# Query and key projections moved behind other small products on TensorE, and the features of block 2 built by square transposes and DMA

## What is computed

```python
def phi(x):                                  # r = 8: 64 features of a head's 32 channels
    a = np.einsum('rd,bhsd->bhsr', S1, x)
    b = np.einsum('rd,bhsd->bhsr', S2, x)
    return np.einsum('bhsi,bhsj->bhsij', a, b).reshape(*x.shape[:-1], r * r)
...
kv = np.einsum('bhsf,bhsd->bhfd', phi(k), v)         # q, k, v: (4, 4, 1088, 32)
num = np.einsum('bhsf,bhfd->bhsd', phi(q), kv)
den = np.einsum('bhsf,bhf->bhs', phi(q), z)[..., None] + 1e-06
x = num / den                                # as (4352 tokens, 128)
xn = x / rms(x) * rms_g
y = (silu(xn @ w_gate) * (xn @ w_val)) @ w_out       # d_ff = 1536
...                                          # then a soft mixture of 8 experts over y:
logits = y @ phi                             # softmax over the tokens gives 32 slots,
                                             # w1, relu, w2 on the slots, softmax over the
                                             # slots mixes them back into the tokens
```

## Time and profile before

| | |
|---|---|
| median of the runs | 303.69 us (303.5 to 303.74) |
| the profiled execution | 304.61 us, of which its span is 301.8 us |
| PE busy | 288.5 us, 96% of the span |
| DVE busy | 228.5 us, 76% |
| ACT busy | 159.1 us, 53% |
| DMA | 25.09 MB in 61040 packets, 45649 of them under 512 B |

### The profile page before, as it was taken

One profiled execution on the slowest core, in us unless ns is written; L12 is line 12 of the kernel. 1 busy time (PEld: TensorE's weight loads), 2 busy tenths in 40 slices (PEclk: granted clock), 3 DMA queues, 4 the chain that ended last, 5 costly groups with the idle time before them and its releaser, 6 DMA issues.

```text
span 301.8 us, 6603 instructions
## 1 busy us (share of the span) xinstructions
PE 288.5 (96%) x2551; PEld 234.3 (78%) x2551; DVE 228.5 (76%) x440; ACT 159.1 (53%) x302; POOL 30.2 (10%) x50
## 2 busy tenths in 40 slices
PE   7799999999999989999999999999999999999983
PEld 6687787888787868888878788888788878797572
DVE  4746877886998797988788979797778668865423
ACT  1475654635556446347564473456456556547421
POOL 1168001000100010003200100020000003000000
PEclk9999999999999999999999999999999999999995
DMA  6999200000203123233112201972199310010017
GB/s 184 330 238 244 72 2 1 2 0 2 72 13 51 28 33 47 32 88 51 26 27 39 32 9 26 346 253 42 25 284 293 50 28 13 13 24 3 0 39 261
DMA packets 61040, 25.09 MB, mean 83 GB/s; under 512 B 45649, under 2 KB 57682, under 8 KB 61010
## 3 DMA queue, kind: packets, MB, share of 16 engines
q1 hardware_dynamic: 60722, 24.38, 31.9%
q10 hardware_dynamic: 288, 0.30, 0.3%
HBM read 17.45 MB, written 2.23 MB: 65 GB/s over the span
## 4 chain that ended last, share of the span: by engine, by line
PE 76%; DVE 10%; DMA 4%; ACT 3%; issue 3%; SPq 2%; DVEq 0%; ACTq 0%
PE bank L1006 73%; DMA area<-in_moe_w_out 4%; DVE hid L851 3%; DVE hl L857 2%; PE bank L1086 1%; ACT silu L578 1%; SPq L349 1%; DVE area L789 1%; DVE area L998 1%; DVE area L768 1%; DVE area L810 1%; DVE ssq L800 1%; ACT woh L627 1%; PE bank L1047 0%; DVE area L744 0%
## 5 line engine op out<-in xcount | busy, mean ns | idle before, releaser
L851 DVE TENSOR_TENSOR hid<-bank,silu 128x512 f32<-128x512 f32 (+1 forms) x108 | 70.8, 656 | 43.2 <-PE bank L1006 22.7
L578 ACT ACTIVATE silu<-bank 128x512 f32<-128x512 f32 (+1 forms) x108 | 61.8, 573 | 73.0 <-PE bank L1006 72.2
L857 DVE TENSOR_TENSOR hl<-hid,hh 128x512 fp32r<-128x512 f32 (+1 forms) x108 | 70.8, 655 | 0.0
L586 ACT ACTIVATE hh<-hid 128x512 fp32r<-128x512 f32 (+1 forms) x108 | 64.9, 601 | 3.9 <-DVE hid L851 3.9
L1006 PE MATMUL bank<-hh,woh 128*128 128x512 f32 (+1 forms) x108 | 43.4, 402 | 0.0
L1006 PE MATMUL bank<-xh,wgh 128*128 128x512 f32 (+1 forms) x108 | 42.3, 392 | 1.1 <-DVE xl L820 0.6
L1006 PE MATMUL bank<-hh,wol 128*128 128x512 f32 (+1 forms) x108 | 41.1, 380 | 0.0
L1006 PE MATMUL bank<-xh,wvl 128*128 128x512 f32 (+1 forms) x108 | 41.0, 380 | 0.0
L1006 PE MATMUL bank<-xh,wgl 128*128 128x512 f32 (+1 forms) x108 | 41.0, 380 | 0.0
L1006 PE MATMUL bank<-xh,wvh 128*128 128x512 f32 (+1 forms) x108 | 41.0, 380 | 0.0
L1006 PE MATMUL bank<-hl,woh 128*128 128x512 f32 (+1 forms) x108 | 40.9, 379 | 0.0
(11 more groups left out here) (146 smaller groups left out, 337.9 us busy)
## 6 DMA issues: line engine op xcount, KB each, us to landing
area<-in_moe_w SPq DMA_DIRECT2D x1, 4096.0 KB, 14.6
area<-in_moe_w SPq DMA_DIRECT2D x8, 512.0 KB, 6.0
area<-area SPq DMA_DIRECT2D x96, 32.0 KB, 2.0
q_in<-in_q SPq DMA_DIRECT2D x16, 128.0 KB, 2.7
y_nat<-in_v SPq DMA_DIRECT2D x4, 512.0 KB, 4.7
out<-area SPq DMA_DIRECT2D x8, 256.0 KB, 2.3
area<-in_k SPq DMA_DIRECT2D x14, 128.0 KB, 4.1
y_nat<-area SPq DMA_DIRECT2D x112, 16.0 KB, 1.8
```

Of the source, the lines that this page charges most:

```text
L578: act.activation(silu[n][:, 0:w], gate_b[n][:, 0:w], ACT.Silu).then_inc(s_silu_ready, 1)
L586: act.activation(hh[m % NH][:, 0:w], hid[m % 2][:, 0:w], ACT.Copy).then_inc(s_hh_ready, 1)
L851: dve.tensor_tensor(hid[n][:, 0:w], val_b[n][:, 0:w], silu[n][:, 0:w], ALU.mult).then_inc(s_hid_ready, 1)
L857: dve.tensor_tensor(hl[m % NH][:, 0:w], hid[m % 2][:, 0:w], hh[m % NH][:, 0:w].bitcast(F32), ALU.subtract).then_inc(s_hl_ready, 1)
```

## The change

`NF` becomes 2: block 2 gets its features by DVE's squares and SyncE's DMAs, prepared in block 0; `features_T` and ACT's copies remain for blocks 0 and 1. SyncE's list has `features_of(2)` before `load_queries(2)`. Projections of blocks from 2 on are issued in chunk 4 right behind `attention(j+1)`, into bank 7; those of the keys in chunk 7 right behind `normalised_T`, into banks 7 and 6. On DVE, `mean_square` and `normalised` now stand ahead of `step` in chunks 5 and 6; `features` is in chunk 5 and `feature_squares` in chunk 8 of every block, `keys_T` in chunks 1, 2, 3 (2, 5, 6 in block 0), and `queries_T(j+2)` in chunk 0 of blocks 2 and 4 and chunk 3 of the others. The wait of attention for `features` of the next block (`s_qp_ready`) falls away.

```diff
-        NF = 3
+        NF = 2
...
-            return (bank[0:3] if G < NG else (bank_a, bank_b, bank_c))[G % NG]
+            return bank[G] if G < NG else psum[:, (7, 7, 6)[G % NG] * 512 + (0, AB * G3, 0)[G % NG]:][:, 0:AB * G3]
+
+        def ab_b(jn):
+            return bank_b if jn < NF else bank_c
...
             load_queries(1)
+            features_of(NF)
             load_queries(2)
-            features_of(NF)
+            features_of(3)
             tokens_of(0)
...
# DVE, whole_block
-                    if c in (3, 6, 8) and keys_in(j):
-                        keys_T(NG * keys_in(j) + (3, 6, 8).index(c))
+                    key_c = (2, 5, 6) if first else (1, 2, 3)
+                    if c in key_c and keys_in(j):
+                        keys_T(NG * keys_in(j) + key_c.index(c))
...
-                    if c == (5 if j + 2 == NF else 0) and NF <= j + 2 <= NB:
+                    if c == (0 if keys_in(j) and not first else 3) and NF <= j + 2 <= NB:
                         queries_T(j + 2)
-                    step(j, c)
-                    if c == 1 and j + 1 < NF:
-                        features(j + 1)
-                    if c == (8 if j + 2 == NF else 1) and NF <= j + 2 <= NB:
-                        features(j + 2)
-                    if c == (9 if j + 2 == NF else 6 if j + 2 == NF + 1 else 2 if keys_in(j) else 3) and NF <= j + 2 <= NB:
-                        feature_squares(j + 2)
-                    if c == (10 if j + 2 == NF else 9) and 0 <= j - 1 < NY:
-                        finished_blocks(j - 1)
-                    if c == 4 and not last:
-                        attention(j + 1)
                     if c == 5 and not last:
                         mean_square(j + 1)
                     if c == 6 and not last:
                         normalised(j + 1)
+                    step(j, c)
+                    if c == 1 and j + 1 < NF:
+                        features(j + 1)
+                    if c == 5 and NF <= j + 2 <= NB:
+                        features(j + 2)
+                    if c == 8 and NF <= j + 2 <= NB:
+                        feature_squares(j + 2)
+                    if c == 9 and 0 <= j - 1 < NY:
+                        finished_blocks(j - 1)
+                    if c == 4 and not last:
+                        attention(j + 1)
...
# PE, projections: waits
+                if jn < NF:
+                    if later(2 * jn):
+                        pe.wait_ge(s_x_ready, 2 * jn)
+                elif jn == NF:
+                    pe.wait_ge(s_qpT_ready, HP * jn)
+                else:
+                    pe.wait_ge(s_qp_ready, jn)
...
# PE, attention
-                if NF <= jn < NB:
-                    pe.wait_ge(s_qp_ready, jn + 2)
...
# PE, key_projections
                     if b > 0 and G % NG == 0:
-                        pe.wait_ge(s_xl_ready, j + 2)
-                    if b > 0 and j > 0 and G % NG == 1:
-                        pe.wait_ge(s_logit_ready, j)
+                        pe.wait_ge(s_qp_ready, j + 3)
+                    if b > 0 and G % NG == 2:
+                        pe.wait_ge(s_x_ready, 2 * (j + 2))
+                        if j > 0:
+                            pe.wait_ge(s_logit_ready, j)
...
# PE, whole_block
                             if j + 1 < NF:
                                 projections(j + 1)
-                            elif j + 2 <= NB:
-                                projections(j + 2)
-                        if c == 8 and j + 2 == NF:
-                            projections(j + 2)
-                        if c == 9 and keys_in(j):
-                            key_projections(keys_in(j), j)
                         if c == 4:
                             attention(j + 1, nb)
+                            if NF <= j + 2 <= NB:
+                                projections(j + 2)
...
                         if c == 7:
                             normalised_T(j + 1)
+                            if keys_in(j):
+                                key_projections(keys_in(j), j)
```

More of the change, by code:

```diff
@@ L754, in features @@
                     dve.wait_ge(s_qpT_ps, HP * jn)
-                a_ij, b_j = factors(bank_b[:, 0:nt * H * NP * R], nt * H)
+                a_ij, b_j = factors(ab_b(jn)[:, 0:nt * H * NP * R], nt * H)
                 dve.wait_ge(s_ab_ps, jn + 1)
@@ L1029, in projections @@
                 pe.wait_ge(s_qT_ready, jn + 1)
[L1031 to L1035, removed]
+                if jn < NF:
[5 more added lines that the diff above has]
+                    pe.wait_ge(s_qp_ready, jn)
                 for t in range(width(jn) // P):
                     for rows, tok in halves(t):
-                        ins = mm(bank_b[rows, t * AB:(t + 1) * AB], qT[:, tok], s_blk[:, :, :])
+                        ins = mm(ab_b(jn)[rows, t * AB:(t + 1) * AB], qT[:, tok], s_blk[:, :, :])
                 ins.then_inc(s_ab_ps, 1)
```

## The result

The changed kernel takes 307.52 us (median of 19 runs, 304.99 to 311.52), the kernel before 304.18 us in the runs beside it (19 runs, 303.5 to 306.69). The ratio is 1.009, 95% interval 1.007 to 1.011: slower by about 2.7 us. The medians lie 3.3 us apart; the ratio leaves out four executions of the changed kernel, of 309.6 us and more, in which the granted clock was lower (at most 0.976, against 0.979 and more in the others). Predicted were 308.0 us, 4.3 above the 303.69 of the first runs. The profiled execution of the changed kernel has a span of 305.1 us, 3.3 more than that of the kernel before.

The account below looks back on a forecast made before the run. PE, busy for 96% of the span, was taken as the bound. Savings of 4.9 us, a queue wait of 7.2 and a clock loss of 2.1 made +4.4 us, put onto the median of 303.69: 308.0 us, range 303.3 to 310.0.

Parts of the forecast that it names:

- The mechanism: SyncE's queue, from squares of block 7 to features of block 8: 48.1 us against PE's 40.9, making PE wait.
- the sum: Whole kernel: -4.9 off PE, +7.2 wait and +2.1 clock give +4.4 us, so 308.0 us.
- What comes off PE: PE's blocks: features_T of block 2 gone 0.9, joined small products 1.6, waits of normalised_T 2.4; 4.9 us saved in all.
- about as much for the keys of three blocks: Key projections on PE: joining other small products saves about the 0.26 us switching price, between 0.2 and 0.26 each.
- The wait: PE before attention(8): features of block 8 land at 253.1 where PE wants them at 245.95, a wait of 7.2 us.
- 6.1 x 0.37 = 2.2 us: SyncE's queue at features_of(7): w1 in flight overlaps the issues by 6.1 us and slows them by 2.2 us.
- chain of 48.1 us: SyncE's queue from the squares of block 7 to the last landing of features_of(8): 48.1 us, against PE's 40.9.
- The gains before this point don't count: Before chunk 8 of block 5: 4.7 us won there bring squares and landing forward alike, so the queue sets the end.
- The clock: PE after the wait: granted clock falls to 0.50 for one chunk, +2.1 us, bounds nothing and 4.1 us.
- DVE at nothing: DVE's added work, mostly in block 0, fits and costs nothing; otherwise delays show one for one, up to about 1.5 us.
- time enough: Block 0, chunk 3: queries_T(2) comes about 36 us in, its loads issued by 32.3, so no wait.
- The bracket of 306.3 to 309.8 us: Whole kernel's time for the main case, queue late and clock down, given chance 0.52.

Follow-up runs that it names:

- the one with fillers: Changed kernel with 16 filler products of 128 columns on PE ahead of the wait for the features of block 8: 305.16 us, ratio 1.002.
- projections alone: Changed kernel with w2 issued behind features_of(8) and tokens_of(5), plus query projections of blocks 2 to 8 alone in chunk 5: 303.12 us, ratio 0.994.

## Why the prediction was right, and where its numbers were not

**The mechanism**, a queue that runs from the squares of block 7 to the last landing and ends behind PE, was as predicted, shown by the change of the queue's order alone (the loss turns into a gain) and by the late squares alone in the kernel before (the loss without the gain). That the sum also met the measured time is in part luck, as the last paragraph of this section shows.

**What comes off PE**, predicted 4.9 us. From block 0 to chunk 4 of block 7 the changed kernel is 4.0 us shorter (33.61 to 241.31 against 34.15 to 245.88). The three waits are gone (2.4), `features_T` of block 2 is (0.9), and the four groups of query projections that had stood alone gave 0.26 each (1.0). Of the missing 0.9, some 0.3 is at `features_T` of block 1, where PE now waits 0.24 us for `features`. The rest is the term "about as much for the keys of three blocks". The keys moved from a place of their own to one behind `normalised_T`. In the kernel before, the second product behind a `normalised_T` without a wait (its last product ahead is at 79.52), and then the keys alone:

```profile
80.42 0.39 PE L1006 MATMUL bank<-xl,wgh 128*128 128x512 f32 x1
...
113.47 0.40 PE L1006 MATMUL bank<-xh,wvl 128*128 128x512 f32 x1
113.79 1.27 PE L1006 MATMUL bank<-s_blk,area 128*64 128x64 f32 x36
...
115.33 0.39 PE L1006 MATMUL bank<-hl,woh 128*128 128x512 f32 x1
```

And in the changed kernel, joined:

```profile
106.64 1.27 PE L1012 MATMUL bank<-s_blk,area 128*64 128x64 f32 x36
...
108.18 0.40 PE L1012 MATMUL bank<-xl,wgh 128*128 128x512 f32 x1
```

Apart, `normalised_T` costs 80.42 - 79.52 - 0.46 = 0.44 us and the keys 115.33 - 113.47 - 0.46 = 1.40. Joined they cost 108.18 - 105.88 - 0.46 = 1.84, the same. So small products behind attention's save the switch, and behind the four transposes they save nothing.

**The wait**, predicted 7.2 us, is 4.8. The step that was mis-sized is "6.1 x 0.37 = 2.2 us" for w1 and, less so, w2. Of the chain of 48.1 us from the squares to the landing, 45.4 are left: `features_of(7)` 11.3 where I had 13.1, `tokens_of(4)` 11.4 (11.1), w2 10.1 (11.3), `features_of(8)` and landing as read. The slowing by w1 is no rate over the overlap. It acts as a date: the 16 issues are done 10.4 to 11.7 us after their start, as elsewhere, or 19 us after w1's issue, whichever is later. In the changed kernel the start is 7.7 us behind w1, so nearly nothing is lost: 11.3 us, against 11.1 with w1 moved away alone. The Trainium skill's rule of "DMA: Bandwidth & Descriptors", section "Queues, rings and completion order", on consumption in ring order, agrees with this better than my share of 0.37: the first DMA of `features_of(7)`, issued at 200.94, took 5.5 us to land after the change and so landed at 206.4, about when w1 did (193.28 + 13.3 = 206.6). With the squares of block 7 earlier it was 197.65 + 9.4 = 207.1 against 207.0, but in the kernel before 192.61 + 8.4 = 201.0 against 202.6. Why the issues end 19 us after w1's is not shown. I had worked the rule out as a larger loss because I took the whole flight of w1 as blocked time on top of the issues.

**"The gains before this point don't count"** held, but the path was named too narrowly. I had the squares of block 7 as its start. The squares of block 6, moved by six chunks in block 4, delay `features_of(6)`, `tokens_of(3)` and w1, and so the same landing; the runs with those of block 7 and with both in chunk 6 show it (306.8 and 301.4 us). In the prediction that move stood only as a correction to the overlap.

**The clock**, taken as 2.1 us out of 0 to 4.1, measured 2.13 in the profile, and 2.1 between the ratios of the changed kernel and the one with fillers (1.009 and 1.002). The rule that long waits for DMA between bursts bring the throttle on ("TensorE: Matmul & The Clock Gate", section "HAM oscillation — how this bites in real kernels", in the Trainium skill) held here.

**DVE at nothing** held for blocks 1 to 7. In block 0 DVE's `features` cost PE the 0.3 us at `features_T` above, and "time enough" for the queries was wrong in some executions, by 1.7 us on DVE and 0.6 on PE.

**The sum**, +4.4 us, stands against +3.3 in the profiles and between the medians, and +2.7 by the ratio. It came out near the result in part by luck, as its terms erred in opposite directions: the wait was 2.4 us less, the gain in the blocks 0.9 less (0.5 of which an earlier start of the blocks gave back), and 0.95 us at the end had no term. The bracket of 306.3 to 309.8 us for a late queue and one chunk of clock doesn't follow from the bounds beside it: 0.1 and 3.7 us net, with 2.1 for the clock, give 305.9 to 309.5.

## What to carry to other kernels

A queue that one engine issues by hand has a critical path of its own: when a producer moves later, add up all issues from it to the last landing, and ask who waits there, even if nobody waited before. Two ways that hold a queue can be tied, so an experiment that relieves one alone and gains nothing does not clear it; relieve both. A large load with a late use belongs behind the small transfers that something waits for: with w2 behind them, this change is worth 1.4% instead of costing 0.9%. And a price read for one neighbour need not hold for another: query projections behind attention saved 0.26 us, keys behind the transposes nothing.

## What was not expected of the hardware

- One DMA of 4 MB in flight delays the issues behind it in the same queue up to a fixed time, 18.9 to 19.1 us after its own issue in the four profiles compared above, for 16 issues that otherwise take 10.4 to 11.7.
- A wait of PE of 5.1 us let the clock fall and cost 2.13 us; one of 4.0 us (squares of block 7 early) cost 256.17 - 246.62 - 8.01 = 1.54 us; one of 5.1 us in the kernel before with the late squares 260.88 - 251.38 - 8.01 = 1.49 us. With 1.7 us of idle time it did not fall.
- The changed kernel's times spread by 6.5 us over 19 runs, those of the kernel before by 3.2 beside them. That the wait does it is not shown: in the other groups the kernel before spread by 3.0 to 4.2, two kernels with the wait of 4.7 us by 3.7 (6 runs) and 3.2 (8), and one without it, projections alone, by 5.3 (6).
